# One small identity product among the first scores, six ahead of the first hidden product, and other places for weight splits, states and a mask in the first chunk

## The reference, cut to what matters

```python
for t in range(S):
    state = alpha[:, :, t, :, None] * state + np.einsum('bhd,bhe->bhde', k[:, :, t], v[:, :, t])
    y[:, :, t] = np.einsum('bhd,bhde->bhe', q[:, :, t], state)
...
h = x @ w_in            # 384 -> 2048
x = (h * np.cos(h)) @ w_out
...
h = np.maximum(np.maximum(x @ w1, x @ w2), x @ w3)    # 384 -> 768
return (h @ w_out).astype(np.float32)
```

## Time and profile before

| | before |
|---|---|
| median of 3 runs | 842.2 us (842.09 to 842.33) |
| profiled execution | 843.79 us |
| its span | 842.1 us |
| TensorE busy | 823.2 us, 98% |
| VectorE busy | 582.0 us, 69% |
| ScalarE busy | 428.0 us, 51% |
| GpSimd busy | 245.7 us, 29% |

### The profile page before, as it was taken

How to read it: one execution, slowest core, us unless ns; L and a number is a source line. 1 busy time by engine, 2 the same in 40 slices (tenths; PEclk the granted TensorE clock), 3 DMA queues, 4 the chain that set the end, 5 groups by cost and what they waited for, 6 DMA issues and landing times.

```text
span 842.1 us, 15514 instructions
## 1 busy us (share of the span) xinstructions
PE 823.2 (98%) x5446; PEld 757.6 (90%) x5446; DVE 582.0 (69%) x1080; ACT 428.0 (51%) x933; POOL 245.7 (29%) x272
## 2 busy tenths in 40 slices
PE   5899999999999999999999999999999999999998
PEld 5789998888888888888888888899999999999998
DVE  7797776877687767776874477676664655665554
ACT  4887775444554454445544456554343534334333
POOL 7886673444244425432442133200000000000000
PEclk9999999999999999999999999999999999999999
DMA  8832432322042204211312002210111010100001
GB/s 240 262 110 62 110 78 74 87 58 58 29 123 57 58 29 122 59 52 35 94 67 76 7 35 72 94 57 1 39 39 38 39 39 37 37 35 3 1 39 38
DMA packets 13778, 54.48 MB, mean 65 GB/s; under 512 B 1968, under 2 KB 2480, under 8 KB 13712
## 3 DMA queue, kind: packets, MB, share of 16 engines
q1 hardware_dynamic: 12992, 49.70, 20.6%
q0 software_dynamic: 720, 3.93, 1.2%
HBM read 44.19 MB, written 9.44 MB: 64 GB/s over the span
## 4 chain that ended last, share of the span: by engine, by line
PE 95%; DVE 2%; ACT 2%; issue 1%; ACTq 0%; DVEq 0%
PE h_ps L1293 7%; PE h_ps L1295 7%; PE h_ps L1294 7%; PE acc_pair L1293 5%; PE acc_pair L1294 5%; PE acc_pair L1295 5%; PE h_ps L1399 4%; PE score L1399 4%; PE h_ps L1401 4%; PE h_ps L1400 4%; PE score L1401 4%; PE score L1400 4%; PE acc_last L1293 3%; PE acc_last L1295 3%; PE acc_last L1294 3%; PE score L1257 3%
## 5 line engine op out<-in xcount | busy, mean ns | idle before, releaser
L463 POOL TENSOR_TENSOR work<-work 128x512 f32<-128x512 f32 (+1 forms) x90 | 119.5, 1328 | 278.8 <-DVE work L993 261.6
L635 ACT ACTIVATE work<-work 128x512 f32<-128x512 f32 (+1 forms) x112 | 63.7, 569 | 136.6 <-POOL work L463 123.0
L1293 PE MATMUL h_ps<-x_hi,w_hi 128*128 128x512 f32 (+1 forms) x282 | 111.3, 395 | 1.8 <-DVE x_lo L929 1.5
L979 DVE TENSOR_TENSOR work<-work,h_ps 128x512 f32<-128x512 f32 (+1 forms) x94 | 58.6, 623 | 67.3 <-ACT work L635 66.6
L1295 PE MATMUL h_ps<-x_lo,w_hi 128*128 128x512 f32 (+1 forms) x282 | 104.3, 370 | 0.0
L1294 PE MATMUL h_ps<-x_hi,w_lo 128*128 128x512 f32 (+1 forms) x282 | 103.5, 367 | 0.0
L871 DVE RECIPROCAL inv_decay<-decay 112x128 f32<-112x128 f32 x96 | 89.6, 942 | 0.5
L642 ACT ACTIVATE g_hi<-work 128x512 fp32r<-128x512 f32 (+1 forms) x112 | 63.5, 567 | 43.0 <-DVE work L979 41.7
L1293 PE MATMUL acc_pair<-g_hi,w_hi 128*128 128x512 f32 (+1 forms) x224 | 81.7, 365 | 0.1
L1295 PE MATMUL acc_pair<-g_lo,w_hi 128*128 128x512 f32 (+1 forms) x224 | 80.4, 359 | 0.0
L1294 PE MATMUL acc_pair<-g_hi,w_lo 128*128 128x512 f32 (+1 forms) x224 | 80.4, 359 | 0.0
(11 more groups left out here) (232 smaller groups left out, 2402.2 us busy)
## 6 DMA issues: line engine op xcount, KB each, us to landing
v_all<-val SPq DMA_DIRECT2D x24, 576.0 KB, 3.7
raw<-qka SPq DMA_DIRECT2D x46, 291.0 KB, 4.6
block_out<-x SPq DMA_DIRECT2D x6, 768.0 KB, 6.0
x_in<-block_out SPq DMA_DIRECT2D x6, 768.0 KB, 4.3
raw<-wb SPq DMA_DIRECT2D x12, 384.0 KB, 3.2
out<-raw POOLq DMA_DIRECT2D x5, 768.0 KB, 3.5
stage_own<-wa SPq DMA_DIRECT2D x6, 384.0 KB, 7.7
x<-wa SPq DMA_DIRECT2D x6, 384.0 KB, 7.0
```

Of the source, the lines that this page charges most:

```text
L463: nc.gpsimd.tensor_tensor(frac[:, cols], turns[:, cols], whole[:, cols], ALU.subtract).then_inc(S["frac_done"], 1)
L635: nc.scalar.activation(cosine[:, cols], frac[:, cols], ACT.Sin, scale=-TURN if half and t < POOL_FRAC else TURN).then_inc(S["cos_done"], 1)
L979: nc.vector.tensor_tensor(gated[:, cols], cosine[:, cols], h, ALU.mult).then_inc(S["g_done"], 1)
L1293: mm(ps, w_hi[:, w_at], xh, start=first, stop=False, skip_group_check=shared)
```

## The change

On TensorE a product of the identity with itself (112 x 112, written to the first hidden bank, its result is never read) is issued once between the scores of units 1 and 2, and six times after unit 7, ahead of the first `hidden1`. On ScalarE `first_state` of units 8 to 15 moves from ahead of the next tile's `turn` to behind the `cosines` of the tile of its outputs, and `high_weights` of tiles 9 to 15 move one tile later each. On VectorE the low weights of tiles 8, 9 and 11 are done in tiles 6, 7 and 9 instead of 5, 6 and 7, and the mask of unit 8 stands ahead of tile 5's `fraction` instead of behind it.

```diff
--- before.py
+++ after.py
@@ -668,8 +668,6 @@
                     x_high0(2)
                 if last:
                     x_high0(3)
-                if i - 1 in OUTPUT_AT and not last:
-                    first_state(OUTPUT_AT[i - 1])
                 turn(i, True)
                 if i == 1:
                     g_high(0, True)
@@ -679,14 +677,13 @@
                 if i in (3, 8, 14):
                     split_keys(*{3: (0, 2), 8: (0, 3), 14: (1, 0)}[i])
                 cosines(i, True)
-                if 0 < i < 5:
+                if i in OUTPUT_AT:
+                    first_state(OUTPUT_AT[i])
+                if 0 < i < TILES1 - 4:
                     high_weights(4 + i)
                 if i in (1, 2, 3):
                     g_high(i, True)
-                if 3 < i and 5 + i < TILES1:
-                    high_weights(5 + i)
             g_high(TILES1 - 1, True)
-            first_state(UNITS - 1)
 
             def split_high(t, s, part):
 
@@ -1008,16 +1005,18 @@
             ahead0 = {**{i: (0, 2, 2 + i) for i in range(2)}, **{i + 3: (0, 3, i) for i in range(4)},
                       **{i + 8: (1, 0, i) for i in range(4)}, **{i + 13: (1, 1, i) for i in range(3)}}
             scan0 = {8: (1, 0), 10: (1, 1)}
-            low0 = {1: (5,), 5: (8,), 6: (9,), 7: (10, 11)}
+            low0 = {1: (5,), 6: (8,), 7: (9, 10), 9: (11,)}
             for i in range(TILES1):
                 if i == 10:
                     x_low0(2)
                 if i == TILES1 - 1:
                     x_low0(3)
+                if i == 5:
+                    mask_scores(0, SCORE_AT[i])
                 fraction(i, True)
                 if i in scan0:
                     scan(*scan0[i])
-                if i in SCORE_AT:
+                if i in SCORE_AT and i != 5:
                     mask_scores(0, SCORE_AT[i])
                 early = i and i not in scan0 and i not in SCORE_AT
                 if i in ahead0 and early:
@@ -1335,12 +1334,20 @@
 
             pe.wait_ge(S["init_pool"], 1)
             pe.wait_ge(S["split_pads"], 2)
+            def identity_products(n):
+
+                for _ in range(n):
+                    mm(h_ps[0][0:ROWS, 0:ROWS], ident[0:ROWS], ident[0:ROWS], start=True, stop=True)
+
             def unit0(u):
                 outputs(0, u)
                 increment(0, u)
 
-            for u in range(4):
-                stage1(0, u)
+            stage1(0, 0)
+            stage1(0, 1)
+            identity_products(1)
+            stage1(0, 2)
+            stage1(0, 3)
             for u in range(3):
                 unit0(u)
             stage1(0, 4)
@@ -1351,6 +1358,7 @@
             stage1(0, 7)
             for u in range(5, FIRST_UNITS):
                 unit0(u)
+            identity_products(6)
             first_tokens, second_tokens = slice(0, HTOK), slice(HTOK, TOK)
             for i in range(TILES1):
                 hidden1(i, i, 0, first_tokens, True)
```

## The result

| | before | after |
|---|---|---|
| median | 842.15 us (842.09 to 842.33, 4 runs) | 852.54 us (851.63 to 853.99, 4 runs) |
| ratio after/before | | 1.0123 (1.0107 to 1.0139) |
| profiled execution | 843.79 us | 853.99 us |

The change makes the kernel slower by 10.4 us, 1.2%. The forecast was 840.1 us, with 838.9 to 841.8 as its range: wrong in sign and in size.

The account below looks back on a forecast made before the run. TensorE, busy 823.2 of 842.1 us, was taken as the bound, with only the opening to win. Parts 1 and 2 (-1.4) plus part 3 (-0.7) gave -2.1 us: 840.1 us from the 842.2 median, range 838.9 to 841.8.

Parts of the forecast that it names:

- are TensorE work that nothing in this change touches: From about 48 us on: the last 790 us of TensorE work are untouched and can only start sooner or later.
- gap of 1.47 us: TensorE's idling ahead of the first hidden product at 24.55: the six products lie in it and cost 0.
- Taken at 0; where that cover failed it would cost the 1 to 2 us.: Moved high_weights delay GpSimd's low halves 12 to 15 and SP's loads 14, 15: cost 0, or 1 to 2 us uncovered.
- rival C: Tile 11: VectorE's low_weights(11) does not come forward, its product is 0.6 us later; 842.8 us, chance 0.06.
- `first_state(15)`: Unit 15's state copies ahead of the last x copies, 0.42 us together: taken at 0, bounds -0.15 and +0.4.
- Part 1: One product between second and third scores fills a 0.36 us break; clock rises at some 15.6 us, gaining 1.2 us.
- rival A: Opening: the clock does not rise earlier; parts 2 and 3 still gain, -0.85 us, 841.3 us; chance 0.30.
- The third listed failure: Opening: the forecast is wrong if the clock's rise depends on when the kernel starts.
- Part 2: Six products ahead of the first hidden product prevent the second clock fall; cost 0, gain 0.2 us.
- the 0.19: ScalarE's turn of tile 0: it came 0.19 us after the tile was free, so preventing the clock's fall gains that.
- Part 3: ScalarE and VectorE orders in tiles 4 to 15: 2.0 us earlier, 1.3 left after tile 8, 0.7 after tile 11.
- TensorE's second fall of the clock: Grant of 0.50 from 26 to 28 us after 1.47 us idling; avoiding it gains 0.19 us, not 1.7.

Follow-up runs that it names:

- both losses mended: After whole (orders and seven products), with TensorE's last-layer loop at slot 0 and GpSimd's low halves spread over later tiles: 842.97 us against 842.82 for before.
- the products with the loop at slot 0: Before with the seven identity products alone and TensorE's last-layer loop at slot 0 of a block: 843.16 us against 843.04 for before.
- slot 236: Before with only the head of TensorE's last-layer loop placed at slot 236 of a 256-instruction block: 849.7 us against 843.04 for before.
- the low half of 15 moved: After without the seven products, GpSimd's low_weights(15) moved from tile 11 to tile 12: 843.56 us against 843.04 for before.
- the halves spread: After without products, GpSimd's low halves 12 and 13 in tiles 8 and 9, 14 in 11, 15 starting 12: 843.07 us against 842.82 for before.
- the low halves back: After without products, VectorE's low weights 8, 9 and 11 back in tiles 5, 6 and 7: 845.98 us against 842.82 for before.
- slot 220: Before with only the head of TensorE's last-layer loop placed at slot 220 of a 256-instruction block: 843.17 us against 843.02 for before.
- the orders alone: After without the seven identity products, keeping the changed ScalarE and VectorE orders: 846.97 us against 843.02 for before.
- after with the loop at slot 0: After with TensorE's last-layer loop put at slot 0 of a block: 846.97 us against 843.02 for before.
- `high_weights` back: After without products, ScalarE's high_weights of tiles 9 to 15 back where before has them: 846.41 us against 843.04 for before.
- the early states and the mask alone: Before with only first_state behind the cosines and unit 8's mask ahead of tile 5's fraction: 842.79 us against 842.82 for before.

## Why the prediction was wrong, point by point

**The sum left out a term.** It said that the last 790 us "are TensorE work that nothing in this change touches", which "can only start sooner or later". That step failed: 6.8 of the 10.2 us arose there. The seven products were costed as time in a gap of 1.47 us, and in that gap they cost nothing, as said (the runs of both losses mended, and of the products with the loop at slot 0). That they are also 28 instructions in TensorE's program (14 matmuls and 14 weight loads in the earlier trace rows against the page of after), hundreds of microseconds ahead of the loop that they move, was in no term and in no rival. The runs put it at 6.7 us by itself (slot 236). Before's packets were to be read in advance: the queue's line and the fact that no packet comes in the second pass say that the loop fits; nothing says by how much.

**"Taken at 0; where that cover failed it would cost the 1 to 2 us."** The moved `high_weights` and GpSimd's low halves were taken at 0. This is the step that failed in the opening, and the loss has three parts. GpSimd waited 1.85 us for the high half of tile 12, from there ran late (a `g_lo` of 2.27 us, a `w_lo` of 3.07), and TensorE's output product of tile 9 waited 0.93 us for it: 1.2 us of the 1.3 left at tile 11 were gone:

```profile
51.55 2.12 POOL L453 TENSOR_TENSOR w_lo<-stage_own,w_hi 128x256 fp32r<-128x256 f32 x3 [1.85 <-ACT w_hi L557]
53.62 2.27 POOL L471 TENSOR_TENSOR g_lo<-work,g_hi 128x256 fp32r<-128x256 f32 x1
55.85 3.07 POOL L453 TENSOR_TENSOR w_lo<-stage_own,w_hi 128x256 fp32r<-128x256 f32 x3
60.95 0.39 PE L1292 MATMUL acc_pair<-g_hi,w_hi 128*128 128x256 f32 x1 [0.93 <-POOL g_lo L471]
```

Then `to_mid` took 3.54 us beside GpSimd's row, and TensorE fell back by 2.1 us; and behind the wait that this made the clock fell, 1.9 us. That the place of GpSimd's low halves decides about the last two is shown by the runs (the low half of 15 moved, the halves spread). That GpSimd's instructions hold `to_mid` is argued from the times at which they end together; GpSimd's row is without pause there in before too, so the row alone isn't the reason. I had thought of GpSimd as late or not late, not as an engine that can slow another's instruction here. That VectorE and GpSimd slow each other was in rival C, for one `low_weights`; C's place (tile 11) fell: that product came 1.3 us earlier, and putting the low halves back mended at most 1 us.

**`first_state(15)`, taken at 0 with bounds of -0.15 and +0.4.** With both losses mended it seems to delay the low part of g of tile 14, and 0.56 us of the lead go there: a little beyond the bound. It was not tested by itself.

**Part 1, -1.2 us.** The first hidden product came at 23.98, 0.57 us earlier and not 1.2. The wait of 0.36 us was filled as said, and the third score came at 11.78, against 11.77. But the clock rose near 16.9 us, not 15.6: of the units the one at 15.94 is still slow and the one at 17.54 quick.

```profile
11.41 0.58 PE L1340 MATMUL h_ps<-ident 112*112 112x112 f32 x2
...
15.94 0.64 PE L1271 MATMUL y_ps<-scores,v_all 128*96 128x128 f32 x2
...
17.54 0.39 PE L1271 MATMUL y_ps<-scores,v_all 128*96 128x128 f32 x2
...
22.34 1.36 PE L1340 MATMUL h_ps<-ident 112*112 112x112 f32 x12
23.98 0.35 PE L1292 MATMUL h_ps<-x_hi,w_hi 128*128 128x256 f32 x1 [0.28 <-DVE x_lo L926]
```

Neither the forecast nor rival A is borne out: over the fourteen profiled executions the rise lies from about 14 to 17 us with the product (five), and from 14 to 18 without (nine), and the first hidden product starts from 23.27 to 23.98 with it and from 23.20 to 24.55 without, before's being the last. So none of the 0.57 can be put down to the product. The third listed failure ("if the clock's rise depends on when the kernel starts") is nearest. "TensorE: Matmul & The Clock Gate" of the Trainium skill, Part 1, says that the place of the rise varies from run to run; the traces agree, by these 4 us. I had set that sentence aside because three times lay within 0.24 us. That was no argument: the profiled execution, the one that I worked from, stood 1.6 us above their median. An early rise is kept, too: in the run of slot 220 it is 1.0 us at the first hidden product and 1.1 at the end. The 65 runs of before beside the experiments point the same way: the 34 whose mean granted clock is 1.00 took 842.8 us in the median, the 24 with 0.998, which the profiled one has, 843.6. So part 1 seems to have won back a late rise that belonged to this one execution, and the sum then took off the 1.6 us between it and the median as well. (The working also has four units and two scores between 15.6 and 18.1 us; the trace of before has one and a half units and one score there. Half of that stretch is what it can save all the same.) Part 4 of that page, on transposes, these runs don't decide.

**Part 2, six products for +0.2 us.** The price was right: they took 1.36 us inside the gap, and the grant stays at 1.00 from 24 to 28 where it was 0.50 from 26 on the earlier trace rows:

```profile
24.00:26.00 2.00, 1.73 (x12) 1.00 0.98 177
26.00:28.00 2.00, 2.00 (x17) 1.00 1.01 402
```

ScalarE's `turn` of tile 0 started at 26.11, 0.74 us earlier, which is 0.57 and 0.17: the 0.19 was right. That it is the products which keep the clock up is likely and not shown: all five profiled executions with them keep it, but so do three of the nine without (slot 236, the low half of 15 moved, the halves spread).

**Part 3 up to tile 11.** Right. With the 1.4 us of the opening it said 3.4 us for the score of unit 10, 2.7 for tile 8's product and 2.1 for tile 11's; take off the 0.65 that the opening fell short, and 2.75, 2.05 and 1.45 stand against 2.79, 2.02 and 1.27 measured. TensorE was waiting for VectorE's low halves ahead of both (1.4 us in two waits, in after's list; 0.5 to 0.8 each was said, 0.6 and 0.83 came). The working holds to 57 us and ended there, with the next step taken at 0; the loss stands at 62 us.

**The clock as a price.** The working put a price on TensorE's second fall of the clock, but to no new wait. In after both long waits that arose were followed by one: 1.9 us lost behind 2.16 of idling, 2.4 behind the 4.4 in the last layer, so that a wait cost one and a half times to twice itself. It is no rule: the same 2.16 us were followed by a fall in two of four profiled executions (after and the orders alone) and by none in two (after with the loop at slot 0, the low halves back).

## What to carry to other kernels

Adding instructions to an engine moves all code behind them, and where a long loop on that engine nearly fills what its instruction memory holds, a few dozen can make it fetch the loop again; compare the packets of the instruction queue before and after, look for waits on "issue" at a loop's second pass, and test by moving the loop's head alone. When work is moved by a tile, follow it on every engine that it wakes, and look for small VectorE instructions that have become long beside GpSimd's. And read a gain far along the chain, not where it arises: here 2.8 us at 47 us were worth nothing at the end, even with both losses mended. Before a lead of a microsecond in one profiled execution is believed or forecast, look at how far two executions of the same program lie apart (here 1.1 us between before and before with its loop at slot 220, most of it from the clock's rise).

## What the runs showed of the hardware that I had not expected

**Instruction fetch.** A packet of instructions is 16 KB (0.77 MB in 47). In after's second pass nine are fetched, just ahead of its first matmul and then at matmuls 5, 42, 128, 255, 378, 498, 598 and 709 of 738. A pass takes 96 us and has 738 matmuls, as many weight loads and 112 other instructions in the trace. The second one runs without any fetch where the loop's head is at slot 0 or 220, and fetches nine packets where it is at 236. "Runtime: NRT & Kernel Launch" of the Trainium skill, "Instruction fetch mechanics", gives 256 instructions for a block and 2048 for what TensorE holds, first in, first out. The trace agrees with the block: at slot 236 twenty slots of it are left, and the second gap stands behind nine matmuls and their nine loads. With 1588 instructions the pass ends in its seventh block at slot 0, and in its eighth at 220 and at 236 alike. What differs between these two is that at 236 a packet comes 28 matmuls before the jump back, and at 220 none in the last 114. That such a packet comes isn't enough: at slot 0 one comes there too, and nothing follows. Eight blocks held would fit the three (seven and the packet, eight without it, eight and the packet, which then takes the place of the first); this is argued from three places, and how many blocks are held wasn't measured. The page calls the crossing of a block's boundary mostly hidden, and says that a taken branch to a target outside the current two pages must wait for its fetch. Here such a wait was 3.1 to 3.5 us at the jump, the next boundary 1.2 to 2.0 us and not hidden, and the clock over 2 us more. But at slots 0 and 220 the jump over these 1588 instructions waited for nothing, so two pages aren't the bound here.

**VectorE beside GpSimd.** A VectorE instruction on 112 x 4 numbers took 0.10, 0.15, 0.52, 0.54, 0.77, 1.47 and 3.54 us in different kernels, and a copy of one tile 3.53. "SBUF — State Buffer" of the Trainium skill says that on the port which VectorE and GpSimd share the second to issue blocks until the first has finished. The traces agree with a block but not with its length: 3.54 us go through five GpSimd instructions, from the first `w_lo` (61.56) into the second (64.33). In before GpSimd ran without pause too, and `to_mid` got through after 0.54 us; with the low half of 15 moved after 1.47, at the same joint of `w_lo` and `g_lo`. Nor is it where in GpSimd's row VectorE arrives: with `high_weights` back it came 0.03 us ahead of the second part of the same `w_lo`, as in after, and was done in 0.10. What lets it in at one joint and not at another stays open, and so do the six slower runs with `high_weights` back, the two with the low halves spread and the one with the early states and the mask alone.
